# Moving the end-of-chunk keys, the state's decay and the first weights' low halves from POOL to VectorE

## The chip, the cores and the metric

The kernel runs on one core of a Trainium2 chip. Its engines work side by side, each through its own list of instructions in order, and meet at semaphores: TensorE (PE, matmuls into PSUM banks), VectorE (DVE), ScalarE (ACT), GpSimd (POOL) and SyncE (SP, which only issues DMAs here). The metric is the device time of one execution in microseconds.

## What is computed

The reference is a gated linear recurrence followed by two MLPs, all in fp32:

```python
for t in range(S):                      # B=4, H=8, S=768, D=48
    S_re, S_im = a_n[t] * (S_re, S_im)  # complex decay, magnitude capped at 0.999
    S_re = S_re + einsum('bhd,bhe->bhde', k[t], v[t])
    y[t] = einsum('bhd,bhde->bhe', q[t], S_re)
x = y as (3072 tokens, 384)
x = relu(x @ w_in)**2 @ w_out                      # MLP1, width 2048
x = (silu(x @ w_gate) * (x @ w_val)) @ w_out2      # MLP2, width 1536
```

## The kernel before

**Tiling.** The recurrence works in chunks of 128 time steps with all 8 heads, 24 chunks; three chunks (384 tokens) make a unit, 8 units. A chunk's steps are: logs and phases of the gates (`magnitudes`, `log_gates`, `phases`), running sums of them on PE (`gate_sums`, `phase_sums`), exponentials and sines on ACT (`decays` gives fF, fG, fE; `sines` gives trig), products into the rotated queries Qn, keys Kn and end-of-chunk keys En, transposes of Qn and Kn on PE (L1152, L1164), evacuated by ACT as QT0 and KT0 (L577, L580), then a hierarchy of block scores (8, 16, 32, 64 steps) whose factors DVE multiplies into QT and KT (`to_borders...`) and whose results it puts into AT. `outputs` forms y from AT and v and from QT and the state St; `state` adds En's product with v to St, after St has been decayed over the chunk.

**Precision.** Large matmuls run as three fp32r products of high and low halves. The high half is a rounding copy on ACT, the low half the difference. MLP1's activations have ghi on ACT (L634) and glo on POOL (`low`, L455); its weights come by DMA into one of two staging buffers, get their high halves on ACT and their low halves on POOL (`weight1`, L450), in seven pieces, three of 2048 and four of 1536 columns. Gates and phases have lnrho_lo, theta_lo and carry_lo on DVE.

**Order.** Every engine's order is written out by hand. The MLP1 work of the two units before is dealt into 11 slots per chunk (`WORKS`, `PLACES`): PE runs it between the pieces of the recurrence, ACT does the ReLU, square and ghi of each (L628 to L634). The last of PE's pieces in a chunk are, in order: `outputs(n)`, `phase_sums(n+1)`, `state(n)`, two slots, `transposes_Q(n+1)`, a slot, `transposes_K(n+1)` and a slot. `transposes_K` has two halves; the second writes bank 2 and waits for it:

```python
pe.wait_ge(ev["sadd"], n - 1)        # DVE's addition to St has read the bank
pe.wait_ge(ev["QTev"], 2 * n - 1)    # ACT has evacuated QT's first part
```

On ACT, a chunk ends with sines(n+1), squares(n+2), slots 7 and 8, evac_QK(n+1) and slots 9 and 10. In the first chunk of units 2 to 7 slot 7 or 8 has `evac_acc` (y1s, L640). DVE ends a chunk with to_start(n), scale_qk(n+1), phases, low_theta, wrap(n+1), rotate(n+1) (Qn L876, Kn L879), low_carry(n+1) (L861), state(n) (L956), msq(n+2) (L796, L798), and opens the next with to_borders (L899), which waits for ACT's DT (L583). Where the chunk opens a unit, `clear_state` (keep L962, St L965) goes first.

POOL's list per chunk in the kernel before is: weight pieces in the first unit, the glo of slots 0 to 6, `decay_state(n)` (L443), `k_end(n+1)` (fE times k, L434; En, L438), the glo of slots 7 to 10. It runs these beside DVE. SP loads the next weight piece when s_wlo says that a staging buffer is free, and the next q and k when DVE's kG and POOL's kE are done.

**Units.** Unit 0 has no MLP work and loads the weights; unit 1 has only MLP work of unit 0; units 2 to 6 are a counted loop, one copy of code; unit 7 follows, then the rest of MLP1, then MLP2 in 8 units, in which POOL does nothing.

Of the kernel before, what the change touches and what calls it, by code (L numbers as in the profile page):

```python
# [27 lines left out]
F32 = mybir.dt.float32  # L28
# [43 lines left out]
def build(nc, gates, qk, v, H, w_in, w_out, w_gate, w_val, w_out2, mats, masks, out):  # L72

    B, S, HD = v.shape
    D = HD // H
# [20 lines left out]
    with top:  # L96
# [139 lines left out]
        def twice(x):  # L236

            return bc(x[:, :].rearrange("p (h a d) -> p h a d", h=H, a=1), [P, H, 2, D])
# [31 lines left out]
        def staged(st, i, dims):  # L270
            x = st[:, i % 2, 0:int(np.prod(dims))]
            return x if len(dims) == 1 else x.rearrange("p (j m) -> p j m", j=dims[0])
# [150 lines left out]
        @block.gpsimd  # L423
        def _(pool):
            for x in (Qn, Kn, En, AT, Dn, St):
                pool.memset(x[:, :, :], 0.0).then_inc(s_init, 1)
            pool.memset(keep[:, :], 1.0).then_inc(s_init, 1)
            pool.memset(half_pi[:, :], math.pi / 2).then_inc(s_init, 1)

            def k_end(n):  # L430

                pool.wait_ge(ev["expE"], n)
                pool.wait_ge(s_qk, 16 * n)
                pool.tensor_tensor(fE[:, :], fE[:, :], k_sb, ALU.mult).then_inc(ev["kE"], 1)  # L434
                pool.wait_ge(ev["kE"], n)
                pool.wait_ge(ev["trig"], n)
                pool.wait_ge(ev["pS"], n - 1)
                pool.tensor_tensor(parts(En), twice(fE), trig[:, :, :, :], ALU.mult).then_inc(ev["En"], 1)  # L438

            def decay_state(n):  # L440
                pool.wait_ge(ev["t128"], n)
                pool.wait_ge(ev["pY"], n)
                pool.tensor_tensor(St[:, :, :], St[:, :, :],  # L443
                                   bc(T128[:, :].rearrange("p (h a) -> p h a", a=1), [KR, H, D]), ALU.mult)\
                    .then_inc(ev["sdec"], 1)

            def weight1(i):
                src, hi, lo, dims = PIECES1[i]
                pool.wait_ge(s_whi, i + 1)
                pool.tensor_tensor(lo, staged(stage1, i, dims), hi.bitcast(F32), ALU.subtract).then_inc(s_wlo, 1)  # L450

            def low(base, j):

                pool.wait_ge(mlp1["hi"], base + j + 1)
                pool.tensor_tensor(glo[:, j % GR, :], rg[:, j % 2, :], ghi[:, j % GR, :].bitcast(F32), ALU.subtract)\  # L455
                    .then_inc(mlp1["lo"], 1)

            def works(ci, slots, u, has_tail, has_head):
                for slot in slots:
                    ws, unit_no = dealt(ci, slot, u, has_tail, has_head)  # L460
                    for kind, j in ws:
                        if kind == "up":
                            low(unit_no * NF1, j)

            def unit(u, has_tail=True, has_head=True, has_next=True):
                flags = (u, has_tail, has_head)
                for ci in range(CPU):
                    n = u * CPU + ci + 1
                    nxt = has_next or ci < CPU - 1
                    pieces = [] if has_head else IN_CHUNK[ci]  # L470
                    for i in pieces[0:2]:
                        weight1(i)
                    works(ci, range(7), *flags)
                    decay_state(n)
                    if nxt:
                        k_end(n + 1)
                    for i in pieces[2:3]:
                        weight1(i)
                    works(ci, (7, 8, 9, 10), *flags)

            pool.wait_ge(s_init, 8)
            k_end(1)
            unit(0, False, False)
            unit(1, False)
            with pool.Fori(2, NU - 1) as u:
                unit(u)
            unit(NU - 1, has_next=False)
            for kind, j in WORKS[HEAD:]:
                if kind == "up":
                    low((NU - 2) * NF1, j)  # L490
            for j in range(NF1):
                low((NU - 1) * NF1, j)
# [299 lines left out]
        def _(dve):  # L792
# [33 lines left out]
            def low_gates(n):  # L826
                dve.wait_ge(ev["lrhi"], n)
                dve.tensor_tensor(lnrho_lo[:, :], lnrho[:, :], lnrho_hi[:, :].bitcast(F32), ALU.subtract).then_inc(ev["lrlo"], 1)
# [20 lines left out]
            def wrap(n):  # L849

                dve.wait_ge(ev["pTheta"], n)
                dve.tensor_scalar(t6[:, :], NAT(0), -1.0, MAGIC, ALU.mult, ALU.add).then_inc(ev["kk"], 1)
                dve.wait_ge(ev["kk"], n)
                dve.wait_ge(ev["cyhi"], n - 1)
                dve.wait_ge(ev["sinw"], n - 1)
                dve.scalar_tensor_tensor(thw[:, :], t6[:, :], MAGIC, NAT(0), ALU.subtract, ALU.add)\
                    .then_inc(ev["thw"], 1)

            def low_carry(n):
                dve.wait_ge(ev["cyhi"], n)  # L860
                dve.tensor_tensor(carry_lo, thw[CARRY:P, :], carry_hi.bitcast(F32), ALU.subtract)\  # L861
                    .then_inc(ev["cylo"], 1)

            def scale_qk(n):
                dve.wait_ge(s_qk, 16 * n)
                dve.wait_ge(ev["expF"], n)
                dve.tensor_tensor(fF[:, :], fF[:, :], q_sb, ALU.mult).then_inc(ev["qF"], 1)
                dve.wait_ge(ev["expG"], n)
                dve.tensor_tensor(fG[:, :], fG[:, :], k_sb, ALU.mult).then_inc(ev["kG"], 1)

            def rotate(n):
# [6 lines left out]
                dve.wait_ge(ev["pKT"], 2 * (n - 1))  # L878
                dve.tensor_tensor(parts(Kn), twice(fG), trig[:, :, :, :], ALU.mult).then_inc(ev["Kn"], 1)  # L879

            def tree8(n):

                dve.wait_ge(ev["pY"], n - 1)
                dve.wait_ge(ev["p0"], n)
                dve.tensor_tensor(T8[:, :], DT[:, :, 0], DT[:, :, 1], ALU.mult).then_inc(ev["t8"], 1)
# [91 lines left out]
            def unit(u, has_tail=True, has_head=True, has_next=True):  # L977
                for ci in range(CPU):
                    c = u * CPU + ci
                    n = c + 1  # L980
                    nxt = has_next or ci < CPU - 1
                    if ci == 0:
                        clear_state(u, c)
                    to_borders(n)
                    if nxt and not has_head:
                        capped(n + 1)
                        denominator(n + 1)
                        log_gates(n + 1)
                        low_gates(n + 1)
                    tree8(n)  # L990
                    in_block(n)
                    tree(n, T16, T8, ev["t8"], ev["t16"])
                    tree(n, T32, T16, ev["t16"], ev["t32"])
                    if nxt and has_head:
                        capped(n + 1)
                        denominator(n + 1)
                        log_gates(n + 1)
                    to_borders16(n)
                    if nxt and has_head:
                        low_gates(n + 1)  # L1000
                    neighbours8(n)
                    if nxt:
                        ratio(n + 1)
                        sides(n + 1)
                    to_borders32(n)
                    neighbours16(n)
                    tree(n, T64, T32, ev["t32"], ev["t64"])
                    tree(n, T128, T64, ev["t64"], ev["t128"])
                    to_borders64(n)
                    if ci == 0 and has_head:  # L1010
                        split_x(u - 1)
                    if not has_head:
                        phases(n + 1)
                        low_theta(n + 1)
                    to_start(n)
                    if nxt:
                        scale_qk(n + 1)
                    if nxt and has_head:
                        phases(n + 1)
                        low_theta(n + 1)  # L1020
                    if nxt:
                        wrap(n + 1)
                        rotate(n + 1)
                        low_carry(n + 1)
                    state(n)
                    if has_next or ci < CPU - 2:
                        msq(n + 2)


            dve.wait_ge(s_const, 48)  # L1030
# [16 lines left out]
            wrap(1)  # L1047
            dve.wait_ge(s_init, 8)
            scale_qk(1)
            rotate(1)  # L1050
            low_carry(1)
            msq(2)
            unit(0, False, False)
            unit(1, False)
# [383 lines left out]
```

## Time and profile before

| what | value |
|---|---|
| median of 3 runs | 1377.71 us |
| lowest to highest run | 1376.91 to 1381.43 us |
| profiled execution, first to last instruction | 1378.7 us |
| mean granted TensorE clock | 0.957 of full |
| DVE busy, whole span | 777.4 us (56%) |
| ACT busy | 758.1 us (55%) |
| POOL busy | 291.5 us (21%) |

The profiled execution has no time of its own beside its span; the span is set against the runs. Busy shares are averages over stages: the recurrence with MLP1 fills the first part of the span, MLP2 the rest. A group of the profile (engine, line, tile, shape) gives the number of its instructions, their busy time and the mean duration of one; in a timeline a row is one instruction or several merged ones, with its start, its duration and in brackets the idle time of its engine before it and whom it waited for. Rows of pipelined instructions overlap, so the distance from one start to the next is often shorter than the duration.

### The profile page before, as it was taken

Reading aid. Unit: us, or ns where it says so; the run is one execution under the profiler, and the core shown is the slowest. Engines: PE = TensorE matmul, PEld = TensorE weight load, DVE = VectorE, ACT = ScalarE, POOL = GpSimd, SP = SyncE. Lnnn points to the kernel's source line nnn. Section 1 sums busy time; section 2 is a strip of 40 time slices with the busy share of each in tenths; the row PEclk is TensorE's granted clock in tenths of the full one; section 3 lists DMA queues with packets and bytes.
Section 4 is the critical chain, followed back from the end, with each engine's and each line's share of the span. In section 5 each row is a group of like instructions: output and inputs, shape, how many; then the busy total and the mean of one; then the engine's idle time right before and its main releaser. Section 6 shows DMA issues by size and latency. Waiting matters only on the chain.

```text
span 1378.7 us, 26842 instructions
## 1 busy us (share of the span) xinstructions
PE 1246.0 (90%) x10390; PEld 1160.4 (84%) x10390; DVE 777.4 (56%) x1221; ACT 758.1 (55%) x1473; POOL 291.5 (21%) x219
## 2 busy tenths in 40 slices
PE   3566799998998998998999998999999999999998
PEld 2455688887887887887888888999999999999998
DVE  5888677877777776777778871125223222232222
ACT  5666677877877776876777764563222222222221
POOL 2533233333333332333333332210000000000000
PEclk9956799999999999999999999899999999999999
DMA  3222111111111111111111102122001000000000
GB/s 130 89 84 73 35 36 53 53 36 54 53 36 53 52 36 53 53 36 53 53 36 52 53 7 66 72 99 81 18 18 35 1 35 17 17 34 1 18 18 18
DMA packets 42139, 62.56 MB, mean 45 GB/s; under 512 B 3120, under 2 KB 37680, under 8 KB 41648
## 3 DMA queue, kind: packets, MB, share of 16 engines
q1 hardware_dynamic: 42032, 60.98, 14.0%
q8 instruction: 86, 1.41, 0.4%
q14 instruction: 21, 0.17, 0.0%
HBM read 46.81 MB, written 14.16 MB: 44 GB/s over the span
## 4 chain that ended last, share of the span: by engine, by line
PE 57%; DVE 27%; issue 9%; ACT 5%; DVEq 0%; ACTq 0%
PE bank L1338 7%; PE bank L1337 7%; PE bank L1336 7%; DVE Kn L879 4%; PE bank L1359 4%; PE bank L1357 4%; PE bank L1355 4%; PE bank L1244 3%; PE bank L1246 2%; PE bank L1245 2%; PE bank L1257 2%; DVE carry L861 2%; PE bank L1261 2%; PE bank L1259 2%; PE bank L1177 2%
## 5 line engine op out<-in xcount | busy, mean ns | idle before, releaser
L455 POOL TENSOR_TENSOR glo<-rg,ghi 128x384 fp32r<-128x384 f32 x128 | 153.6, 1200 | 486.4 <-ACT ghi L634 486.4
L1072 DVE TENSOR_TENSOR prod<-bank,silu 128x384 f32<-128x384 f32 x96 | 53.5, 557 | 285.7 <-PE bank L1338 269.3
L742 ACT ACTIVATE silu<-bank 128x384 f32<-128x384 f32 x84 | 41.5, 494 | 281.0 <-PE bank L1338 281.0
L1244 PE MATMUL bank<-xhi,win_hi 128*128 128x384 f32 x384 | 141.8, 369 | 8.7 <-DVE xlo L974 7.2
L1257 PE MATMUL bank<-ghi,wout_hi 128*128 128x384 f32 x384 | 135.7, 353 | 0.0
L1246 PE MATMUL bank<-xhi,win_lo 128*128 128x384 f32 x384 | 133.4, 348 | 0.0
L1245 PE MATMUL bank<-xlo,win_hi 128*128 128x384 f32 x384 | 133.0, 346 | 0.0
L1261 PE MATMUL bank<-ghi,wout_lo 128*128 128x384 f32 x384 | 129.8, 338 | 0.0
L1177 PEld LDWEIGHTS bank<-QT,KT 112*64 112x64 f32 x2304 | 84.8, 156 | 53.3 <-issue 26.4
L1259 PE MATMUL bank<-glo,wout_hi 128*128 128x384 f32 x384 | 129.4, 337 | 0.0
L1177 PE MATMUL bank<-QT,KT 112*64 112x64 f32 x2304 | 95.4, 244 | 34.7 <-issue 13.8
L628 ACT ACTIVATE rg<-bank 128x384 f32<-128x384 f32 x128 | 62.7, 489 | 100.8 <-PE bank L1246 99.8
L1359 PE MATMUL bank<-p_hi,wo_lo 128*128 128x384 f32 x288 | 96.2, 334 | 0.0
L1357 PE MATMUL bank<-p_lo,wo_hi 128*128 128x384 f32 x288 | 96.2, 334 | 0.0
L1355 PE MATMUL bank<-p_hi,wo_hi 128*128 128x384 f32 x288 | 96.2, 334 | 0.0
L1244 PEld LDWEIGHTS bank<-xhi,win_hi 128*128 128x128 f32 x384 | 75.3, 196 | 13.6 <-issue 5.8
L747 ACT ACTIVATE p_hi<-prod 128x384 fp32r<-128x384 f32 x96 | 50.2, 523 | 51.2 <-DVE prod L1072 32.4
L1245 PEld LDWEIGHTS bank<-xlo,win_hi 128*128 128x128 f32 x384 | 75.9, 198 | 0.0
L1246 PEld LDWEIGHTS bank<-xhi,win_lo 128*128 128x128 f32 x384 | 75.4, 196 | 0.0
L1257 PEld LDWEIGHTS bank<-ghi,wout_hi 128*128 128x128 f32 x384 | 72.7, 189 | 2.7
L1259 PEld LDWEIGHTS bank<-glo,wout_hi 128*128 128x128 f32 x384 | 72.8, 190 | 0.0
L1261 PEld LDWEIGHTS bank<-ghi,wout_lo 128*128 128x128 f32 x384 | 72.6, 189 | 0.0
(162 smaller groups left out, 3207.3 us busy)
## 6 DMA issues: line engine op xcount, KB each, us to landing
gates_sb<-in_gates SPq DMA_DIRECT2D x48, 192.0 KB, 2.4
qk_sb<-in_qk SPq DMA_DIRECT2D x24, 384.0 KB, 3.1
v_sb<-in_v SPq DMA_DIRECT2D x24, 192.0 KB, 3.2
xT_scratch<-yT SPq DMA_DIRECT2D x48, 96.0 KB, 2.9
xin<-xT_scratch SPq DMA_DIRECT2D x8, 576.0 KB, 4.1
y1T_scratch<-y1s SPq DMA_DIRECT2D x8, 576.0 KB, 3.5
x<-y1T_scratch SPq DMA_DIRECT2D x8, 576.0 KB, 4.0
out<-o_sb SPq DMA_DIRECT2D x8, 576.0 KB, 2.9
```

The costliest lines, as they stand in the source:

```text
L455: pool.tensor_tensor(glo[:, j % GR, :], rg[:, j % 2, :], ghi[:, j % GR, :].bitcast(F32), ALU.subtract)\
L1177: ins = nc.tensor.matmul(banks[bank][rows, h * HALF:(h + 1) * HALF], k[:, h, rows], q[:, h, rows], start=True, stop=True)
L1244: nc.tensor.matmul(banks[4][:, 0:UT], win_hi[:, k, c], xhi[:, k, :], start=k == 0, stop=False)
L1245: nc.tensor.matmul(banks[4][:, 0:UT], win_hi[:, k, c], xlo[:, k, :], start=False, stop=False)
L1246: ins = nc.tensor.matmul(banks[4][:, 0:UT], win_lo[:, k, c], xhi[:, k, :], start=False, stop=k == KT3 - 1)
L1257: nc.tensor.matmul(dst, wout_hi[:, j, c], ghi[:, j % GR, :], start=j == 0, stop=False, skip_group_check=True)
L1259: nc.tensor.matmul(dst, wout_hi[:, j, c], glo[:, j % GR, :], start=False, stop=False, skip_group_check=True)
L1261: ins = nc.tensor.matmul(dst, wout_lo[:, j, c], ghi[:, j % GR, :], start=False, stop=j == NF1 - 1, skip_group_check=True)
L1336: nc.tensor.matmul(dst, hi[:, k, c], xh[:, k, :], start=k == 0, stop=False)
L1355: nc.tensor.matmul(dst, wo_hi[:, j, c], p_hi[:, j % GR, :], start=j == 0, stop=False, skip_group_check=True)
L1357: nc.tensor.matmul(dst, wo_hi[:, j, c], p_lo[:, j % GR, :], start=False, stop=False, skip_group_check=True)
L1359: ins = nc.tensor.matmul(dst, wo_lo[:, j, c], p_hi[:, j % GR, :], start=False, stop=j == NF2 - 1, skip_group_check=True)
```

## The change

`k_end`, `decay_state` and `weight1` leave POOL's list, which keeps `low` alone. On DVE they stand as follows: `k_end(n+1)`, now only fE times k, behind scale_qk(n+1); `decay_state(n)` between low_carry(n+1) and state(n); En as a function of its own, `rotate_end(n+1)`, as the last of the chunk; a weight piece ahead of tree8(n), one between wrap(n+1) and rotate(n+1), one behind state(n), all in unit 0 alone. ACT, PE and SP are as they were.

```diff
@@ block.gpsimd: k_end, decay_state and weight1 are deleted
-                    for i in pieces[0:2]:
-                        weight1(i)
-                    works(ci, range(7), *flags)
-                    decay_state(n)
-                    if nxt:
-                        k_end(n + 1)
-                    for i in pieces[2:3]:
-                        weight1(i)
-                    works(ci, (7, 8, 9, 10), *flags)
-
-            pool.wait_ge(s_init, 8)
-            k_end(1)
-            unit(0, False, False)
+                    works(ci, range(SLOTS), *flags)
@@ block.vector: the same functions, with En apart
+            def k_end(n):
+
+                dve.wait_ge(ev["expE"], n)
+                dve.wait_ge(s_qk, 16 * n)
+                dve.tensor_tensor(fE[:, :], fE[:, :], k_sb, ALU.mult).then_inc(ev["kE"], 1)
+
+            def rotate_end(n):
+
+                dve.wait_ge(ev["kE"], n)
+                dve.wait_ge(ev["trig"], n)
+                dve.wait_ge(ev["pS"], n - 1)
+                dve.tensor_tensor(parts(En), twice(fE), trig[:, :, :, :], ALU.mult).then_inc(ev["En"], 1)
...
+                    pieces = [] if has_head else IN_CHUNK[ci]
...
+                    for i in pieces[0:1]:
+                        weight1(i)
                     tree8(n)
...
                     to_start(n)
                     if nxt:
                         scale_qk(n + 1)
+                        k_end(n + 1)
                     if nxt and has_head:
                         phases(n + 1)
                         low_theta(n + 1)
                     if nxt:
                         wrap(n + 1)
+                    for i in pieces[1:2]:
+                        weight1(i)
+                    if nxt:
                         rotate(n + 1)
                         low_carry(n + 1)
+                    decay_state(n)
                     state(n)
+                    for i in pieces[2:3]:
+                        weight1(i)
                     if has_next or ci < CPU - 2:
                         msq(n + 2)
+                    if nxt:
+                        rotate_end(n + 1)
...
             scale_qk(1)
+            k_end(1)
             rotate(1)
             low_carry(1)
+            rotate_end(1)
             msq(2)
```

## Rows read from the trace of the kernel before

**Rows 1.** The page: busy us (share) and count by engine; the chain that ended last, by engine.

```profile
PE 1246.0 (90%) x10390; PEld 1160.4 (84%) x10390; DVE 777.4 (56%) x1221; ACT 758.1 (55%) x1473; POOL 291.5 (21%) x219
...
PE 57%; DVE 27%; issue 9%; ACT 5%; DVEq 0%; ACTq 0%
```

**Rows 2.** Busy time of each engine in three stretches, with TensorE's granted clock.

```profile
core 0: us, PE busy (x) PEld busy (x) DVE busy (x) ACT busy (x) POOL busy (x), PEclk, DMA share, GB/s
...
69.00:94.00 25.00, 13.94 (x154) 10.99 (x154) 20.06 (x35) 14.12 (x25) 6.88 (x2) 0.50 0.15 48
...
572.00:677.00 105.00, 95.60 (x968) 85.61 (x967) 79.58 (x124) 77.95 (x156) 32.88 (x26) 0.97 0.16 47
...
900.00:1378.00 478.00, 473.13 (x2754) 472.30 (x2752) 134.77 (x231) 124.83 (x247) 5.06 (x5) 1.00 0.09 29
```

**Rows 3.** Groups of instructions on DVE, whole span.

```profile
L879 DVE TENSOR_TENSOR Kn<-fG,trig 128x768 f32<-128x768 f32 x24 | 62.2, 2590 | 0.0
...
L876 DVE TENSOR_TENSOR Qn<-fF,trig 128x768 f32<-128x768 f32 x24 | 24.1, 1005 | 51.8 <-ACT trig L568 51.8
...
L869 DVE TENSOR_TENSOR fG<-fG,qk_sb 128x384 f32<-128x384 f32 x24 | 13.3, 552 | 0.0
...
L970 DVE TENSOR_TENSOR wg_lo<-stage,wg_hi 128x1536 fp32r<-128x1536 f32 x3 | 5.3, 1759 | 39.2 <-ACT wg_hi L617 39.2
```

**Rows 4.** Timeline at the end of a second chunk, DVE, then POOL, then PE.

```profile
499.99 0.96 DVE L876 TENSOR_TENSOR Qn<-fF,trig 128x768 f32<-128x768 f32 x1 [2.20 <-ACT trig L568]
...
500.87 2.60 DVE L879 TENSOR_TENSOR Kn<-fG,trig 128x768 f32<-128x768 f32 x1
...
503.50 1.25 DVE L861 TENSOR_TENSOR carry<-thw,carry 32x384 fp32r<-32x384 f32 x1
...
504.78 0.56 DVE L956 TENSOR_TENSOR St<-bank,St 112x384 f32<-112x384 f32 x1
...
507.13 1.22 DVE L899 TENSOR_TENSOR QT<-QT,DT 112x1024 f32<-112x1024 f32 x1 [0.93 <-ACT DT L583]
...
500.09 2.56 POOL L438 TENSOR_TENSOR En<-fE,trig 128x768 f32<-128x768 f32 x1 [1.27 <-ACT trig L568]
...
503.82 0.60 PE L1164 MATMUL bank<-ident,Kn 128*112 128x128 f32 x4
...
505.47 0.65 PE L1164 MATMUL bank<-ident,Kn 128*112 128x128 f32 x4 [1.05 <-DVE St L956]
```

**Rows 5.** Timeline of ACT at the end of a first chunk.

```profile
470.65 1.10 ACT L577 ACTIVATE QT<-bank 112x512 f32<-112x512 f32 x2
...
472.87 0.60 ACT L580 ACTIVATE KT<-bank 112x512 f32<-112x512 f32 x1 [0.64 <-PE bank L1164]
```

**Rows 6.** Timeline of DVE where a chunk opens unit 7.

```profile
750.69 1.23 DVE L899 TENSOR_TENSOR QT<-QT,DT 112x1024 f32<-112x1024 f32 x1 [0.42 <-ACT DT L583]
```

**Rows 7.** Timeline of PE after two turns of the counted loop.

```profile
338.26 1.98 PE L1177 MATMUL bank<-QT,KT 112*64 112x64 f32 x32 [2.77 <-issue]
...
544.83 1.98 PE L1177 MATMUL bank<-QT,KT 112*64 112x64 f32 x32 [4.45 <-issue]
```

**Rows 8.** Timeline of a second chunk: DVE's low_theta, PE's phase sums.

```profile
494.38 0.56 DVE L832 TENSOR_TENSOR theta_r<-theta,t_r 128x384 fp32r<-128x384 f32 x1 [0.59 <-ACT t_r L527]
...
495.45 0.44 PE L1122 MATMUL bank<-t_r,sums_r 128*128 128x384 f32 x1
```

**Rows 9.** Timeline of unit 0: DVE, then ACT, then PE.

```profile
38.07 4.46 DVE L891 TENSOR_TENSOR T<-T 112x64 f32<-112x64 f32 x2
...
64.62 4.30 DVE L796 TENSOR_TENSOR t<-t 128x384 f32<-128x384 f32 x1
...
60.26 1.90 ACT L612 ACTIVATE win_hi<-stage 128x2048 fp32r<-128x2048 f32 x1
...
94.19 3.22 PE L1233 MATMUL bank<-v_sb,En 128*112 128x48 f32 x16
...
132.37 0.65 PE L1164 MATMUL bank<-ident,Kn 128*112 128x128 f32 x4 [2.03 <-DVE St L956]
```

More of the change, by code:

```diff
@@ L428, in _ @@
             pool.memset(half_pi[:, :], math.pi / 2).then_inc(s_init, 1)
[L430 to L450, printed above, removed]
             def low(base, j):
@@ L463, in works, with unit @@
                             low(unit_no * NF1, j)
-            def unit(u, has_tail=True, has_head=True, has_next=True):
+            def unit(u, has_tail=True, has_head=True):
                 flags = (u, has_tail, has_head)
                 for ci in range(CPU):
-                    n = u * CPU + ci + 1
-                    nxt = has_next or ci < CPU - 1
-                    pieces = [] if has_head else IN_CHUNK[ci]
-                    for i in pieces[0:2]:
-                        weight1(i)
-                    works(ci, range(7), *flags)
-                    decay_state(n)
-                    if nxt:
-                        k_end(n + 1)
-                    for i in pieces[2:3]:
-                        weight1(i)
-                    works(ci, (7, 8, 9, 10), *flags)
-            pool.wait_ge(s_init, 8)
-            k_end(1)
-            unit(0, False, False)
+                    works(ci, range(SLOTS), *flags)
             unit(1, False)
@@ L486, in _ @@
                 unit(u)
-            unit(NU - 1, has_next=False)
+            unit(NU - 1)
             for kind, j in WORKS[HEAD:]:
@@ L879, in rotate, with decay_state, weight1 @@
                 dve.tensor_tensor(parts(Kn), twice(fG), trig[:, :, :, :], ALU.mult).then_inc(ev["Kn"], 1)
+            def k_end(n):
[7 more added lines that the diff above has]
+                dve.tensor_tensor(parts(En), twice(fE), trig[:, :, :, :], ALU.mult).then_inc(ev["En"], 1)
+            def decay_state(n):
+                dve.wait_ge(ev["t128"], n)
+                dve.wait_ge(ev["pY"], n)
+                dve.tensor_tensor(St[:, :, :], St[:, :, :],
+                                  bc(T128[:, :].rearrange("p (h a) -> p h a", a=1), [KR, H, D]), ALU.mult)\
+                    .then_inc(ev["sdec"], 1)
+            def weight1(i):
+                src, hi, lo, dims = PIECES1[i]
+                dve.wait_ge(s_whi, i + 1)
+                dve.tensor_tensor(lo, staged(stage1, i, dims), hi.bitcast(F32), ALU.subtract).then_inc(s_wlo, 1)
             def tree8(n):
```

## The prediction

> **What bounds the kernel now.** I began with the busy times and the shares of the chain that ended last [rows 1]. TensorE leads both, but busy TensorE is pipelined matmuls with modelled ends, so I went on to the stretches [rows 2]. From 900 us on TensorE is busy 473 of 478 us: that is MLP2, which the change doesn't touch. Before about 858 us the three engines of the recurrence take turns: in 572 to 677 us DVE works 79.6 of 105 us, ScalarE 78.0, POOL 32.9. So this stage is set by a chain that crosses engines, and a microsecond taken off one engine counts only where the next link waits for it.
>
> The groups by line [rows 3] show the oddity. Qn and Kn are the same DVE instruction on the same shape, 128x768, two SBUF inputs; Qn takes 1005 ns, Kn 2590 ns. The timeline of one chunk's end [rows 4] shows why: POOL's En, also two SBUF inputs of 768, runs from 500.09 to 502.65, and Kn, begun at 500.87, ends at 503.47, 0.8 us after En. carry_lo, 32x384, then takes 1.25 us behind POOL's glo; 384 columns that nothing holds take 0.55 (fG, [rows 3]). What hangs on them is TensorE's second half of the K transposes. It waits for the St addition on DVE: the first half starts at 503.82, the second at 505.47, with 1.05 us idle. From there the chain goes over KT, DT and to_borders into the next chunk.
>
> **The change, part by part.**
>
> *Kn and En.* With En gone from POOL I take Kn at Qn's 0.88 us from start to start (499.99 to 500.87) in place of 2.63: DVE gains 1.75 us per chunk. Bounds: nothing if Kn is slow of itself, 1.75 at most.
>
> *carry_lo.* It comes 1.75 us earlier, ahead of glo, and shrinks from 1.25 to about 0.5. Bounds: 0 to 0.75.
>
> *decay_state on DVE.* 112x384 with two SBUF inputs; nearest row fG, 552 ns, 0.48 from start to start (both 128x384). It stands between carry_lo and St, so it is on the path: minus 0.48 (up to 1.25 if glo holds it, as it held carry_lo).
>
> So St could end 1.75 + 0.75 - 0.48 = 2.0 us earlier. **That is not what the chunk gains.** TensorE runs without a gap up to 503.82, so the first K half cannot move. The second can follow it at 0.58 (0.65 is its last row, pipelined) and not at 1.65: the gain is 1.65 - 0.58 = 1.07 us. The excess, 0.9 us, becomes slack of St. The second half also needs ScalarE's evacuation of QT's first part, which is done by then here.
>
> *First chunk of a unit.* There ScalarE evacuates y1s just before QT [rows 5], QT's two parts run 470.65 to 471.75, and KT part 2 must queue at 472.15 behind QT and KT part 1, against 472.87 now. The gain is 0.72; ScalarE is next in line.
>
> *En at the end of DVE's chunk.* Price 0.96 (Qn's), bounds 0.96 to 2.59 (Kn held). It follows msq, and next is to_borders, which now waits 0.93 us for DT [rows 4]. DVE reaches msq's end 2.0 us sooner, DT comes 1.07 sooner: idle becomes 0.93 + 2.0 - 1.07 = 1.9 us, and En (0.9, or 1.7 if a glo holds msq or it) fits. Hidden; without that cover it would cost 0.9 x 23 = 21 us. Where the next chunk opens a unit, DVE also flips keep and clears St; its wait before to_borders is 0.42 there [rows 6]. There the DVE end decides, gain 0.7. At the four turns of the counted loop this doesn't count: TensorE then stands 2.8 to 4.5 us for "issue" [rows 7], more than DVE lacks. I leave those stalls as they are.
>
> *k_end (fE times k) on DVE.* 0.48 per chunk, ahead of phases. low_theta ends at 494.94, its consumer, the phase sums, starts at 495.45 behind the output matmuls [rows 8]: 0.5 us of slack covers it. In the other chunks high_theta waits in ScalarE's order for a ReLU group anyway. Cost 0; if all were exposed, 23 x 0.48 = 11 us. The wait behind it (expE, qk) is long met; queued behind are phases and wrap. kE comes earlier for SP's next q, k and v loads, which nobody waits for. No DMA is moved; SP's weight loads wait for s_wlo, which comes sooner.
>
> *First unit, weights' low halves.* Now POOL's win_lo and wout_lo hold DVE: T takes 4.46 us for two small instructions, msq's addition 4.30 [rows 9]. On DVE a 128x1536 piece is 1.76 us [rows 3], 128x2048 by columns an estimated 2.35. Piece 0: ScalarE's hi ends about 1.3 us after low_gates, plus 2.25, against the 4.0 lost in T: gain 0.3, and 0.45 from the prologue's K transposes (TensorE ends Qn's there first). Pieces 1, 4 and 6 lie in the 2.2 us in which DVE waits for the sines: 0.1 for the first. Piece 2: DVE waits for hi at 62.16 (60.26 + 1.90), works to about 64.45, then msq and En, to_borders at about 66.25. Now it starts after msq's 64.62 + 4.30 and a short second step, at 69.2: gain 3.0. Pieces 3 and 5 cost 1.67 each and remove 2.5 minus some waiting for hi: minus 0.15 each. The second chunk's end gains nothing: state and transposes run back to back on TensorE at the low clock [rows 2, 9]. The third's second K half waited 2.03 us on St at 132.37, behind a Kn and a carry_lo held by POOL; counted through with St, msq, En and the clearing, DVE reaches to_borders 2.05 us sooner. Unit 0: 0.3 + 0.45 - 0.1 + 3.0 - 0.3 + 2.05 = 5.4.
>
> **Sum.** Chunk ends with a successor in units 1 to 7: first chunks 6 x 0.72 + 1 x 1.07 (unit 1 has no y1s) = 5.4; second chunks 7 x 1.07 = 7.5; third chunks 4 x 1.07 + 2 x 0.7 = 5.7; together 18.6. With unit 0: 24.0. The profiled span is 1378.7 us, so 1354.7; it stands 1.0 above the median of the runs shown (1377.71), so I forecast **1353.7 us**.
>
> A rule against this change: row first, DVE is the busiest of the elementwise engines, 79.6 of 105 us, and it gets 0.48 + 0.48 + 0.96 us more work per chunk while POOL, at 32.9, gives it up [rows 2, 3]. The Trainium skill (Perfetto Trace Analysis, Identifying the Most-Contended Engine) has one optimize the engine of highest occupancy first; loading it further would by that reading cost time, some 24 x 1.9 = 46 us if all of it told. The row of Kn speaks against that reading: part of DVE's occupancy is waiting.
>
> **Rivals.**
> 1. *En lands on the path* (0.10). If glo, now able to overlap decay, msq or En, pushes DVE's end by 0.8 more, to_borders comes later than DT. Then about 0.5 a chunk goes: 24 - 23 x 0.5 = 12.5 gained, 1365. For: glo starts within 0.3 us of ScalarE's ghi, and held carry_lo. Against: 1.9 us of room.
> 2. *Slower: Kn is slow of itself* (0.04). Then En on DVE costs 2.6 as well, and nothing comes back. DVE's end moves by 0.48 + 2.6 - 0.93 = 2.15 us: 23 x 2.15 = 49, 1427. It decides from the point where En and decay together exceed 0.93 idle plus what Kn and carry_lo give back. Against: Qn, equal in shape, at 1005 ns [rows 3].
> 3. *No change* (0.03): TensorE's own stream sets the stage, 95.6 of 105 busy, and fills what is freed: 1377. Against: 1.05 us idle before the second K half, 288 MLP matmuls of a unit at about 0.17 us start to start are only 50 us.
> 4. *More* (0.12). Fewer gaps keep TensorE from the 0.50 clock of 69 to 94 us [rows 2], where the state matmuls took 3.2 us [rows 9] of which the full clock saves up to half, and the loop's stalls shorten from about 4 to the least seen, 2.8: 2 x 1.5 + 4 x 1.2, another 8 us, 1346.
> 5. *It doesn't do what it says*: En, decay and weights leave POOL in the diff's text; none.
>
> The rest, 0.71, is my forecast. The range runs from rival 4 with 2 us beyond (1344) to just short of rival 1 (1363): it leaves out rivals 2 and 3 and most of 1. Within 0.3% (4 us, about what a measurement of this kernel can tell from no change) 0.03, slower 0.04, faster 0.93.
>
> **What would show it.** Right: Kn near 1000 ns and carry_lo near 550; the second K transposes directly behind the first, in first chunks waiting for ScalarE's QT; DVE's wait before to_borders still there, about 1 us, after En; the 4 us T and msq rows of unit 0 gone; MLP2 unchanged. Wrong: Kn still above 2 us; to_borders directly behind En; phase sums waiting for low_theta; longer "issue" stalls at the loop's turns.

## The result, and the profile after

The changed kernel takes **1340.81 us** (median of 4 runs, 1340.01 to 1341.81), the kernel before beside it 1377.31 us (4 runs, 1375.29 to 1381.43): a ratio of 0.9722 with the interval 0.9707 to 0.9737, 36.5 us less. The forecast was 1353.7 with a range of 1344 to 1363: the sign was right, the gain half as large again as predicted, and the time lies below the range. The profiled execution spans 1338.2 us against 1378.7, 40.5 less; I account for that difference and say where the runs differ from it. Two later traces of the same changed kernel (e6, e12 below) span 34.9 and 33.4 us less than the same trace of the kernel before, so what follows is the account of one pair of executions.

The page of the changed kernel, with its parts on busy time and on the chain that ended last:

```profile
PE 1230.1 (92%) x10390; PEld 1149.7 (86%) x10390; DVE 773.1 (58%) x1300; ACT 753.0 (56%) x1473; POOL 162.8 (12%) x140
...
PE 65%; DVE 20%; ACT 7%; issue 7%; DVEq 0%; ACTq 0%
```

DVE has 79 more instructions than in [rows 1]. Its part of the chain fell from 27 to 20%. The stages, by windows of equal work: MLP2 (from 859 us) is unchanged at 478 us, so all of the gain lies ahead of it.

```profile
69.00:94.00 25.00, 16.52 (x162) 13.06 (x162) 22.33 (x40) 15.22 (x27) 0.00 (x0) 0.59 0.19 54
...
859.00:1337.00 478.00, 473.63 (x2757) 472.80 (x2755) 134.69 (x231) 125.19 (x248) 5.05 (x5) 1.00 0.09 28
```

The groups on DVE that answer to [rows 3], and the two that came from POOL:

```profile
L840 DVE TENSOR_TENSOR Qn<-fF,trig 128x768 f32<-128x768 f32 x24 | 23.0, 959 | 45.7 <-ACT trig L532 45.7
L843 DVE TENSOR_TENSOR Kn<-fG,trig 128x768 f32<-128x768 f32 x24 | 22.8, 952 | 0.0
L856 DVE TENSOR_TENSOR En<-fE,trig 128x768 f32<-128x768 f32 x24 | 22.8, 950 | 0.0
...
L862 DVE TENSOR_TENSOR St<-St,T 112x384 f32<-112x384 f32 x24 | 13.4, 558 | 5.2 <-PE bank L1230 4.5
...
L825 DVE TENSOR_TENSOR carry<-thw,carry 32x384 fp32r<-32x384 f32 x24 | 13.3, 554 | 0.7
```

Kn went from 2590 to 952 ns, which gives DVE 24 x 1.64 = 39 us back; with carry_lo and unit 0's T and msq free of POOL too, DVE is busy 4 us less than before although it took on En, fE, the decay and seven weight pieces. What that did to TensorE is in the group of the K transposes, first of the kernel before, then of the changed one (last column: idle time ahead of them and what ended it):

```profile
L1164 PE MATMUL bank<-ident,Kn 128*112 128x128 f32 x192 | 30.9, 287 | 27.3 <-DVE St L956 24.9 <-DVE Kn L879 2.4
```

```profile
L1168 PE MATMUL bank<-ident,Kn 128*112 128x128 f32 x192 | 27.3, 279 | 3.7 <-ACT QT L541 3.2 <-DVE St L946 0.5
```

The wait for St is gone (24.9 to 0.5 us); what remains is a wait for ScalarE's QT, 3.2 us. The end of a second chunk, which answers to [rows 4], on DVE, then POOL, then TensorE:

```profile
479.44 0.95 DVE L843 TENSOR_TENSOR Kn<-fG,trig 128x768 f32<-128x768 f32 x1
480.43 0.56 DVE L825 TENSOR_TENSOR carry<-thw,carry 32x384 fp32r<-32x384 f32 x1
481.02 0.56 DVE L862 TENSOR_TENSOR St<-St,T 112x384 f32<-112x384 f32 x1
481.61 0.56 DVE L946 TENSOR_TENSOR St<-bank,St 112x384 f32<-112x384 f32 x1
482.08 0.55 DVE L760 TENSOR_TENSOR t<-t 128x384 f32<-128x384 f32 x1
482.66 1.04 DVE L762 TENSOR_SCALAR t<-t 128x384 f32<-128x384 f32 x1
483.63 0.94 DVE L856 TENSOR_TENSOR En<-fE,trig 128x768 f32<-128x768 f32 x1
484.50 1.21 DVE L889 TENSOR_TENSOR QT<-QT,DT 112x1024 f32<-112x1024 f32 x1
...
481.81 1.68 POOL L433 TENSOR_TENSOR glo<-rg,ghi 128x384 fp32r<-128x384 f32 x1 [5.73 <-ACT ghi L598]
...
482.39 1.04 PE L1168 MATMUL bank<-ident,Kn 128*112 128x128 f32 x8
483.36 0.62 PE L1172 MATMUL bank<-ident,Dn 32*112 32x32 f32 x8
```

From Kn's start to St's is 2.17 us, where it was 3.91: 1.74 earlier. The eight K transposes run as one row of 1.04 us. And QT starts directly behind En: the cover that En needed is used up here, because the second instruction of msq (L762) took 1.04 us beside glo, where it took 0.36 before. QT starts 0.10 us after ScalarE's DT ends (484.40); where DVE waits for DT it starts 0.03 after. So En is late by 0.06 us in second chunks, and by 0.2 to 0.3 in the third chunks of units 1 to 6.

A turn of the counted loop is the jump from its last instruction back to its first. TensorE's wait there answers to [rows 7]. The waits of TensorE from 300 to 700 us (total, times, longest), before and after:

```profile
PE bank L1177 <- issue: 13.8, 4, 4.5
```

```profile
PE bank L1181 <- issue: 9.0, 4, 2.7
```

```profile
518.28 1.15 PE L1181 MATMUL bank<-QT,KT 112*64 112x64 f32 x32 [1.93 <-issue]
```

Behind the turn at 544.83 of [rows 7] the 32 score matmuls took 1.98 us, at a granted clock of 0.50 (the 1.2 GHz level), behind this one 1.15, at 1.00 (2.4 GHz).

**Where the 40.5 us came from** (each the difference of the distances from one Kn to the next in the two traces): unit 0 with the prologue 8.9; unit 1's first chunk end 2.4; the four stretches over a turn 1.2, 1.8, 4.5 and 4.9, together 12.4 (against the same trace of before, e6 gives 12.5 and e12 7.8); six other first chunk ends at 0.80 to 0.87; six second chunk ends at 1.21 to 1.34; the two third chunk ends without a turn 0.99 and 1.92; together 39.3. The last second chunk end lies behind the last Kn and shows in the span, 1.2.

### The profile page after: what moved, and what is told of

Read it like the earlier page. It is cut to its first block, busy times and chain, and to the rows that moved or that the text cites. A ratio compares the mean times of both kernels' runs of the same rounds, so it can differ in the third digit from the quotient of the medians.

```text
span 1338.2 us, 26822 instructions
## 1 busy us (share of the span) xinstructions
PE 1230.1 (92%) x10390; PEld 1149.7 (86%) x10390; DVE 773.1 (58%) x1300; ACT 753.0 (56%) x1473; POOL 162.8 (12%) x140
## 4 chain that ended last, share of the span: by engine, by line
PE 65%; DVE 20%; ACT 7%; issue 7%; DVEq 0%; ACTq 0%
PE bank L1340 7%; PE bank L1342 7%; PE bank L1341 7%; PE bank L1363 4%; PE bank L1359 4%; PE bank L1361 4%; PE bank L1248 3%; PE bank L1261 3%; PE bank L1250 3%; PE bank L1249 3%; PE bank L1265 3%; PE bank L1263 3%; PE bank L1181 2%; PE bank L1229 2%; PE bank L1230 2%
## 5 line engine op out<-in xcount | busy, mean ns | idle before, releaser
L433 POOL TENSOR_TENSOR glo<-rg,ghi 128x384 fp32r<-128x384 f32 x128 | 157.6, 1232 | 709.7 <-ACT ghi L598 709.7
L1181 PEld LDWEIGHTS bank<-QT,KT 112*64 112x64 f32 x2304 | 80.5, 149 | 51.2 <-DVE KT L907 20.9
L1181 PE MATMUL bank<-QT,KT 112*64 112x64 f32 x2304 | 90.9, 237 | 33.1 <-DVE KT L907 15.4
```

Source lines behind the costliest of these rows:

```text
L1181: ins = nc.tensor.matmul(banks[bank][rows, h * HALF:(h + 1) * HALF], k[:, h, rows], q[:, h, rows], start=True, stop=True)
```

## The experiments

No kernel below leaves out any part of the computation. Ratios are against runs of the kernel before on the same chip. "Turns" is the sum of TensorE's four issue waits at its loop's turn, in one trace.

**The parts, each alone.** First k_end and En on DVE, decay and weights left on POOL:

```diff
@@ block.gpsimd
-                    if nxt:
-                        k_end(n + 1)
@@ block.vector
                         scale_qk(n + 1)
+                        k_end(n + 1)
...
                         msq(n + 2)
+                    if nxt:
+                        rotate_end(n + 1)
```

(the first chunk's k_end and rotate_end move in the same way)

> Only the end-of-chunk keys (fE times k, and En) go to VectorE, the state's decay and the weights' low halves stay on POOL. Theory (Kn and carry_lo were held by En on POOL, and TensorE's second K transposes hung on them): nearly the whole steady gain, some 1.25 us per chunk, so about 1347 to 1352 us; Kn near 950 ns outside unit 0; unit 0 keeps its 4 us rows. Rival (Kn is slow of itself): slower than before, above 1400 us. Rival (the gain came from POOL's shorter list as a whole): about half of it, near 1359 us.

Measured: 1349.16 us (ratio 0.9766, 0.9742 to 0.9789); turns 12.1 us. Kn 1031 ns, En 947 ns. This part alone brings 32 us of the change.

Then only the low halves of MLP1's weights on DVE:

```diff
@@ block.gpsimd
-                    for i in pieces[0:2]:
-                        weight1(i)
@@ block.vector
+                    for i in pieces[0:1]:
+                        weight1(i)
                     tree8(n)
```

(the other pieces where the change has them)

> Only the seven low halves of MLP1's weights go to VectorE. Theory: it acts in unit 0 alone, 4 to 7 us gained against the kernel before (about 1371 to 1373 us), the T row of 4.46 us falls to about 0.45 and Kn stays at 2.6 us. Rival (it also changes TensorE's clock and what follows): 10 us or more.

Measured: 1376.1 us (0.9959, 0.9945 to 0.9972), about 5 us less than the 1381.09 of the kernel before beside it; turns 13.8; Kn stayed at 2592 ns. The two parts add up: 31.9 and 5.0 us, for the 36.5 of the whole.

The changed kernel with decay_state back on POOL:

```diff
@@ block.gpsimd
-                    works(ci, range(SLOTS), *flags)
-
+                    works(ci, range(7), *flags)
+                    decay_state(u * CPU + ci + 1)
+                    works(ci, (7, 8, 9, 10), *flags)
...
@@ block.vector
-                    decay_state(n)
                     state(n)
```

> The changed kernel with the state's decay put back on POOL. Theory (TensorE's first K transposes end the wait, VectorE has 0.9 us to spare there): same as the changed kernel within 3 us, 1338 to 1344 us. Rival (the decay sits on the path): 0.48 us x 23 = 11 us faster, about 1330 us.

Measured: 1342.85 us (0.9715, 0.9691 to 0.9738); turns 12.1. St then ends 0.6 us sooner, and first and second chunk ends gain nothing by it (0.81 to 0.85 and 1.28 to 1.33 us, as in the changed kernel); the two third chunk ends without a turn gain 0.1 to 0.2 more (1.14 and 2.03 us). So decay on DVE is paid from slack, nearly as the prediction had it.

**Is it En's place or En's engine?** The kernel before, with one wait added: En stays on POOL and waits for carry_lo.

```diff
@@ block.gpsimd, k_end
                 pool.wait_ge(ev["trig"], n)
+                pool.wait_ge(ev["cylo"], n)
```

> The kernel before, all work left where it was, but En on POOL also waits for carry_lo's semaphore, so it begins when Kn and carry_lo are done. Theory (what cost was the overlap, not the engine): Kn near 950 ns, and 15 to 28 us gained, about 1350 to 1362 us, a little less than the change because the late En holds msq's addition and the glo behind it. Rival (POOL must be rid of the work): no gain, or slower because En and glo come late.

Measured: 1358.29 us (0.9826, 0.9801 to 0.985). At a third chunk's end of it, DVE and POOL:

```profile
525.75 0.95 DVE L880 TENSOR_TENSOR Kn<-fG,trig 128x768 f32<-128x768 f32 x1
526.74 0.56 DVE L862 TENSOR_TENSOR carry<-thw,carry 32x384 fp32r<-32x384 f32 x1
527.32 0.56 DVE L957 TENSOR_TENSOR St<-bank,St 112x384 f32<-112x384 f32 x1
527.80 0.55 DVE L797 TENSOR_TENSOR t<-t 128x384 f32<-128x384 f32 x1
528.38 1.87 DVE L799 TENSOR_SCALAR t<-t 128x384 f32<-128x384 f32 x1
...
527.52 2.51 POOL L439 TENSOR_TENSOR En<-fE,trig 128x768 f32<-128x768 f32 x1 [5.18 <-DVE carry L862]
```

Nothing but the time at which POOL begins En changed, and Kn fell from 2590 ns to 0.95 us here (mean of all 24, those of unit 0 included, 1151 ns). First and second chunk ends gain 0.82 to 0.87 and 1.27 to 1.33 us, the same as in the changed kernel. So the cause of the steady gain is that Kn and En no longer meet; on which engine En runs does not matter to these two. At third chunk ends it does: the late En holds msq, QT starts 0.5 us later than DT would let it, and the two of them without a turn gain 0.37 and 1.26 us against 0.98 and 1.91. Most of what this kernel lacks against the changed one is at the turns, 18.1 us of waits, and in unit 0.

**The kernel before and the changed one again, and both with the loop of units 2 to 6 written out on all engines.** The edit of the latter on each of the five:

```diff
-            with pe.Fori(2, NU - 1) as u:
+            for u in range(2, NU - 1):
                 unit(u)
```

> The kernel before once more, for a second trace. If TensorE's stall at the four turns of the counted loop is a fixed cost of the code, the four come out as 2.8, 2.7, 4.5 and 3.9 us again; if it depends on where things fall in time, they differ by a microsecond or more from run to run.

> The changed kernel once more, for a second trace. Fixed cost: stalls of 2.7, 2.2, 1.9 and 2.2 us again. Otherwise: others.

> The kernel before with the counted loop over units 2 to 6 of the first stage written out on all engines: no turns. Theory: each of the four turns costs its stall less what the next link waits for anyway, and half-clock matmuls behind it, 2.4 to 4.0 us each: 10 to 16 us faster than before, about 1361 to 1368 us. Rival (the stall hides under other waits): same as before.

> The changed kernel written out in the same way. Theory (the change took 3 to 4 us from each of the two long turns, above what Kn gave back): the turns cost less here, so this gains only 4 to 9 us, about 1332 to 1337 us, and the written-out pair differs by less than the pair with loops: 28 to 33 us instead of 36.5. Rival (turns cost both kernels the same): 10 to 16 us here too, about 1327 us, and the pair differs by 36.

Measured: before again 1379.58 us (one run), turns 13.9, singly 4.31, 2.97, 3.95 and 2.64 where the first trace had 2.77, 2.69, 4.45 and 3.89: the single waits vary from execution to execution; after again 1345.57 (one run), turns 8.8; before written out 1362.39 (0.9868, 0.9849 to 0.9888); after written out **1335.16** (0.968, 0.9659 to 0.9701), the fastest kernel here. The same place as above, in the last:

```profile
511.56 0.62 PE L1172 MATMUL bank<-ident,Dn 32*112 32x32 f32 x8
512.36 1.15 PE L1181 MATMUL bank<-QT,KT 112*64 112x64 f32 x32 [0.18 <-ACT KT L544]
```

No turn, no issue wait. The pair without loops differs by 27.2 us (I had expected 28 to 33), the pair with loops by 36.5: **some 9 us of the gain hang on the four turns.** The size is rough. From the ratios a turn costs the kernel before (1 - 0.9868) x 1379.84 / 4 = 4.6 us (4.4 by the medians) and the changed one (0.9722 - 0.968) x 1379.84 / 4 = 1.4 us, with a ratio taken from the runs of the result and intervals that leave 0.6 to 2.3; the one run of e6 beside the written-out kernel gives 2.6. By these ways the turns' share is 7 to 12 us. Without loops the chunk ends gain 0.79 to 0.85 (first), 1.19 to 1.23 (second), 1.03 to 1.08 (third), and everything up to the fifth Kn, the end of unit 0, 8.4.

**Why is the turn shorter?** Four causes were tried. POOL's own turn and the length of its list:

```diff
@@ block.gpsimd (kernel before; and the same edit in the changed one)
-            with pool.Fori(2, NU - 1) as u:
+            for u in range(2, NU - 1):
```

> The kernel before with POOL's share of the counted loop written out, the other engines' loops as they are: POOL has no turn. Theory (TensorE's stall at a turn is longer when POOL turns at the same time): the four stalls fall from 13.8 us together to about 9, as in the changed kernel, and the time by 5 to 9 us, to about 1371 to 1375 us. Rival (POOL's turn has no part; the state of TensorE's own list decides): stalls near 13.8 us and the same time as before.

> The changed kernel with POOL's share of the loop written out. Theory: POOL's short list adds little, so the stalls fall below 9 us together by at most 2 and the time by at most 3 us. Rival (POOL's turn is what is left of the stall): stalls near 0 and about 1335 us, as with all engines written out.

In the changed kernel, 30 one-column memsets were put into each unit of POOL's loop:

> The changed kernel with ten one-column memsets per chunk added to POOL's list in the looped units, on a tile that nobody reads; they read nothing from SBUF. Theory (the length of POOL's list in the loop, refetched at each turn, lengthens TensorE's stall): the four stalls grow from 9.0 us together to 12 or more, and the time by 4 to 8 us against the changed kernel. Rival (length is nothing, only late work of POOL is): stalls near 9 us, time within 3 us of the changed kernel.

and the changed kernel unedited was timed once more beside them:

> The changed kernel unaltered, timed beside the three kernels above, with a third trace. Theory: 36 to 38 us below the kernel before, stalls of 8.7 to 9.1 us together again. Rival (the stalls are chance): any sum between 8 and 14 us.

Measured: e9 1378.77 us (0.9983, 0.9968 to 0.9999), turns 14.4; e11 1341.72 (0.9715, 0.9688 to 0.9742), turns 9.4; e10 1345.63 (0.9751, 0.973 to 0.9773), turns 8.5; e12 1341.7 (0.9709, 0.9693 to 0.9724), turns 11.4 in its trace. Neither POOL's turn nor its list lengthens the waits. The memsets did cost about 4 us against e12, with intervals that don't overlap, but not at the turns of its trace; where is open. And e12 shows how far chance goes: the unedited changed kernel had 9.0, 8.8 and 11.4 us of waits in three traces, the kernel before 13.8 and 13.9 in two. The load of MLP1's input, which SP issues close to the turn, was held back until the unit's first scores, or done twice:

```diff
@@ block.sync (held)
                     if has_head and ci == 0:
+                        sp.wait_ge(ev["p0"], n)
                         mlp1_load(b_next * 2 - 3 + half)
@@ block.sync (twice)
                 sp.wait_ge(s_xst, 32 * CPU * (u + 1))
+                sp.dma_start(xin[:, :, :], xin_view[:, :, bass.ds(u * UT, UT)]).then_inc(s_dup, 16)
+                sp.wait_ge(s_dup, 16 * (u + 1))
```

> The changed kernel; SyncE issues the load of MLP1's input (576 KB, about 4 us to land) only when TensorE has done the unit's first block of scores, so behind TensorE's turn of the loop. Theory (at a turn TensorE fetches its next instructions behind this load: it resumed 7.2 to 9.4 us after the load's issue in every kernel so far): with no load under way the wait at a turn falls from about 2.2 us to under 1 us, some 5 us in all, unless the late load makes ScalarE's split late. Rival (the length of the turn is fixed by TensorE alone, and the load has no part): 1.9 to 2.9 us each as in the changed kernel, time 1338 to 1346.

> The kernel before with the load of MLP1's input held in the same way. Theory: the waits at its four turns (13.8 us in all) fall to at most those of the changed kernel, under 8 us in all, and the time to about 1368. Rival (the load has no part): 13 to 14.5 us in all and the time as before.

> The changed kernel; the load of MLP1's input is done twice, the second when the first has landed, so that TensorE's turn falls wholly under a load. Theory: TensorE resumes some 4 us later after the first issue (11 to 13 us), and the four waits grow from about 9 to over 20 us. Rival: they stay at 8 to 12 us, and only what waits for the input itself moves.

> The kernel before with the load of MLP1's input done twice. Theory: its four waits grow from 13.8 to over 22 us. Rival: 13 to 14.5 us.

Measured: f1 1340.06 us (0.9716, 0.9686 to 0.9745), turns 10.3; f2 1379.27 (1.0004, 0.9987 to 1.0021), turns 13.8; f3 1339.41 (one run), turns 10.1; f4 1382.73 (one run), turns 15.8. The load is not the cause; my theory fell. Last, TensorE's loop alone kept, those of the four others written out:

> The kernel before with the loops of SyncE, POOL, ScalarE and VectorE written out (units 2 to 6) and TensorE's alone kept. Theory (TensorE's turn is long because several engines turn within a few microseconds and fetch instructions together): its four waits, 13.8 us in all before, fall to about 8 us, and the time to some 1370. Rival (TensorE's turn is long by what surrounds it on TensorE itself): they stay at 13 to 15 us, and the time at 1377 to 1380.

> The changed kernel with TensorE's loop alone kept. Theory: its four waits fall to the same as in the kernel before with TensorE's loop alone, 2 us each or less, time about 1339. Rival: 8.5 to 11 us in all as in the changed kernel, time 1340 to 1345.

Measured: g1 1379.41 us (1.0004, 0.9988 to 1.002), turns 16.4; g2 1343.97 (0.974, 0.9706 to 0.9774), turns 9.0. That theory fell too, and something is gained: with TensorE's loop alone kept neither kernel got faster, so what a turn costs comes from TensorE's own loop.

The DMA view has a queue of instructions, q8. Its packets are 16 KB each, and there are 86 in the kernel before, 84 in the changed one and 78 in either with its loops written out. In g1 and g2 no other engine jumps, so I take the fetches of q8 at a turn as TensorE's. Here they are for the 3 us that hold those of one turn, g1 at 545 to 548 us (TensorE resumes at 550.52), then g2 at 519 to 522 us (it resumes at 523.31); the columns are packets, MB, share of the 16 engines:

```profile
q8 instruction: 2, 0.03, 7.4%
```

```profile
q8 instruction: 1, 0.02, 2.7%
```

Two instruction fetches against one. I took this view in steps of 0.2 us at all 72 turns of the 18 traces with loops, so a time ahead can be up to 0.2 us less than the table has it. What I call close together is a pair at most 1 us apart:

```
                                fetches before TensorE resumes     wait at the turn
kernel before (and e5, e2, e9,  two close together, the first      3.84 to 4.45 us   18 turns
 f2, f4, g1)                     4.2 to 4.8 us ahead
                                one, 2.6 to 3.0 us ahead            2.62 to 3.01 us   10 turns
e3 (En late on POOL)            two close together, 4.4 us ahead    4.26 to 4.80 us    4 turns
e1, e4                          two close together, 4.2 to 4.6      2.85 to 3.24 us    8 turns
changed kernel (and e6, e10,    two close together, 4.2 to 4.6      3.40 to 3.56 us    3 turns
 e11, e12, f1, f3, g2)          one, 2.6 to 3.4 us ahead            1.91 to 2.95 us   29 turns
```

Within each kernel the long waits are those in which TensorE fetches two pieces of its program close together at the turn, and it resumes 4.2 to 4.8 us after the first of them, not 2.6 to 3.4 us after a single one. "Single" is not quite exact: seven of the ten turns in the second line have another fetch 6.6 to 6.8 us ahead, and three of the 29 in the last have one 4.3 to 4.7 us ahead, over 1 us from the next. The changed kernel has the pair at 3 turns of 32, the kernel before and its kin at 18 of 28, e1, e3 and e4 at all.

With equal fetches the changed kernel's wait is about 0.6 us shorter than that of the kernel before. One cause offers itself: the work that lies behind TensorE's last wait and covers the fetch, all eight transposes of K and those of Dn, 1.6 us, where the kernel before has half of K's and Dn's, 1.2 us. It does not hold up. e3 has the same 1.6 us and the longest waits of all:

```profile
528.72 1.04 PE L1165 MATMUL bank<-ident,Kn 128*112 128x128 f32 x8
529.68 0.62 PE L1169 MATMUL bank<-ident,Dn 32*112 32x32 f32 x8
534.72 1.55 PE L1178 MATMUL bank<-QT,KT 112*64 112x64 f32 x24 [4.41 <-issue]
```

With a pair of fetches and 1.6 us of covering work, e1 and e4 wait 2.85 to 3.24 us, the changed kernel 3.40 to 3.56, e3 4.26 to 4.80. What goes with the difference is when the first fetch begins: 1.2 to 1.4 us before TensorE's work ends in e1 and e4, 0.6 to 0.9 before in the changed kernel, and in e3 as it ends or up to 0.5 after. What sets that moment is not known.

The Trainium skill (Runtime: NRT & Kernel Launch, Instruction fetch mechanics) has it that a taken branch to a place outside the window held by the engine forces a DMA fetch of the target before execution goes on; the trace agrees, at 2 to 5 us a turn. What triggers the second fetch, and why less often in the changed kernel, whose list on TensorE is the same, stays open.

## Why the prediction was wrong in size

**Right.** *Kn and En*: Kn fell by 1.64 us a piece, priced at 1.75 from start to start, and e3 shows the cause. St starts 1.74 us sooner behind Kn's start, for the 2.0 of the sum. *carry_lo*: 554 ns. *decay_state*: 558 ns, 0.59 from start to start where 0.48 was priced, and on slack (e4). *k_end*: TensorE's wait for theta_r, in all 24 chunks, went from 9.4 to 9.7 us, so it cost nothing that counts. *First chunk of a unit*: 0.72 predicted, 0.80 to 0.87 measured, with ScalarE's QT next in line as said:

```profile
450.03 1.10 ACT L541 ACTIVATE QT<-bank 112x512 f32<-112x512 f32 x2
...
450.69 0.65 PE L1168 MATMUL bank<-ident,Kn 128*112 128x128 f32 x4 [0.16 <-ACT QT L541]
```

*Second chunk*: 1.07 predicted, 1.2 to 1.34 measured. The eight transposes with no wait in their middle run from 482.39 and Dn follows at 483.36, 0.97 later; I had let the second half begin 0.58 after the first. *Rule against the change*: the Trainium skill's advice to optimize the engine of highest occupancy first (Perfetto Trace Analysis, Identifying the Most-Contended Engine) would by my reading have had DVE's load cost up to 46 us; DVE was given 79 instructions more and its busy time fell from 777.4 to 773.1. The better page of the Trainium skill for this kernel is SBUF — State Buffer (Who interferes with whom): a VectorE instruction with two SBUF inputs contends with a GpSimd instruction that reads SBUF, for ports of which one of them has an exclusive lock at a time; the trace agrees (Kn 2.60 us beside En, 0.95 alone).

**Wrong.** The step that failed is "I leave those stalls as they are", with 1.07 us for each of the four turns. I treated TensorE's issue wait as a fixed piece that only follows the chunk end. It is not fixed: it went from 13.8 to 9.0 us over the four turns. About half of that came from fetches that fell together at two turns before and at none after; why the rest fell is open, as is what sets the fetches. The clock adds to it. In the kernel before, the scores behind all four turns ran at the lower granted clock (1.98 us behind waits of 2.77 and 4.45 alike); in the changed one they took 1.86, 1.52, 1.15 and 1.15 us, behind waits of 2.74, 2.16, 1.93 and 2.15. The traces give 12.4 us over the four turns in place of 4.3: 4.8 from the waits, about 4 from the chunk ends, the rest from the clock. The pairs with and without loops give 7 to 12 us for the turns' own share. Rival 4 had named the waits' shortening (down to 2.8, and the clock, for unit 0), had a chance of 0.12, and was too cautious: the waits went to 1.93. It did not name the reason, the fetches. The range's lower end of 1344 came from that 2.8, "the least seen". That was the least in one trace (the same trace has a 2.69 as well); it was no bound.

**Mis-sized terms.** Against the 24.0 us of the sum, the trace's 40.5 add: the turns 8.1; unit 0 3.5 (8.9 for 5.4); unit 1's first chunk end 1.3 (2.4 for 1.07: the nine MLP1 matmuls between Dn and the scores took 3.1 us from 167.40 us in the kernel before, at a clock of 0.50, and 1.8 us in the changed one, at 1.00); six first chunk ends 0.7; seven second chunk ends 1.4; the two third chunk ends outside a turn 1.5 (their 0.7 each was too little: without loops they gain 1.03 and 1.08). Together 16.5. Without turns the forecast holds better: 24.0 for the 27.2 us of the written-out pair, most of the rest in unit 0.

*Unit 0* term by term. The prologue gave 1.4, not 0.45. Piece 0 gave nothing, not 0.3: it lies whole on the path, but T is free.

```profile
36.24 2.29 DVE L869 TENSOR_TENSOR win_lo<-stage,win_hi 128x2048 fp32r<-128x2048 f32 x1 [1.24 <-ACT win_hi L576]
...
40.15 0.45 DVE L881 TENSOR_TENSOR T<-T 112x64 f32<-112x64 f32 x2
```

Piece 1 gave 1.1 that I had not seen: in the kernel before, POOL's win_lo at 54.22 held Qn, which took 2.06 us where it takes 0.96 now. Up to the third Kn the gain was 4.0 to 4.9 us in the changed kernel's traces, more than the terms' 3.5. From there on it varies: up to the fifth Kn the same kernel gained 8.9, 3.4 and 8.2 us in three executions (after, e6, e12), and the granted clock from 88 to 153 us was 0.70, 0.58 and 0.67 in them. That the clock decides fits these three numbers; no experiment shows it. A gain in so idle a stage is no fixed number.

**What En's cover was worth.** I predicted about 1 us of DVE idle before to_borders, behind En. It is there in first chunks (0.62 us at 452.41); in second and third chunks it is nil, as the timeline shows for a second one. That is one of the signs that the prediction had named for being wrong, "to_borders directly behind En", and the bound of 1.7 us for En "if a glo holds msq" was what happened. It overran the cover by 0.06 us in second chunks and 0.2 to 0.3 in third ones. Rival 1 thus came true in kind, at well under its 0.5 us a chunk.

## What to carry to other kernels

When an instruction takes two and a half times its twin's time on the same shape, look at which other engine's instruction it overlaps; moving either in time can bring most of what moving it to another engine brings, as e3's single wait shows (22.8 us of the 31.9 of e1). Where a counted loop's engine stands for "issue" at the turn, don't carry that wait through as a constant: look at the instruction fetches there, or write the loop out, if the program may grow; here that was worth 17 us before the change and about 6 after it (4 to 10 by the runs at hand). And take the least wait seen in one trace as a sample, not as a bound.

## What the runs showed that was not expected

- TensorE resumes 2.6 to 3.4 us after a single instruction fetch at a loop's turn and 4.2 to 4.8 us after the first of two close together; which of the two it is varies from turn to turn within one execution (the kernel before: 2.77, 2.69, 4.45, 3.89 us).
- Writing out the loops of all engines but TensorE changes nothing (1.0004); writing out TensorE's as well gives 17 us.
- A DVE instruction with one input waits for POOL as well: msq's TENSOR_SCALAR took 1.04 us beside glo and 1.87 us beside En, 0.36 us alone, while the two-input instruction just before it ran in its usual 0.55 us with POOL's already begun. From POOL's side, glo took 1.68 us there and 1.00 us alone. My prediction had counted POOL's hold on msq as a bound, not as what would happen.
